# The bonus term of a linear-attention kernel as four 64x64 matmul tiles, with its results in other PSUM banks

## The reference

```python
for t in range(S):
    kt, vt, rt, wt = (k[:, :, t], v[:, :, t], r[:, :, t], w[:, :, t])
    cur = np.einsum('bhd,bhe->bhde', u[None] * kt, vt)
    y[:, :, t] = np.einsum('bhd,bhde->bhe', rt, state + cur)
    state = wt[:, :, :, None] * state + np.einsum('bhd,bhe->bhde', kt, vt)
```

## Time and profile before

| what | value |
|---|---|
| median of 3 runs | 313.41 us |
| the profiled execution: its time, its span | 313.47 us, 311.8 us |
| TensorE matmul busy | 306.1 us, 98% of the span |
| VectorE, ScalarE, GpSimd busy | 199.5, 160.8, 110.7 us |
| granted TensorE clock, mean | 0.999 |
| chain that ended last, TensorE's share | 98% |

### The profile page before, as it was taken

How to read it: one execution, slowest core, us unless ns; L and a number is a source line. 1 busy time by engine, 2 the same in 40 slices (tenths; PEclk the granted TensorE clock), 3 DMA queues, 4 the chain that set the end, 5 groups by cost and what they waited for, 6 DMA issues and landing times.

```text
span 311.8 us, 7335 instructions
## 1 busy us (share of the span) xinstructions
PE 306.1 (98%) x2882; PEld 290.0 (93%) x2882; DVE 199.5 (64%) x349; ACT 160.8 (52%) x335; POOL 110.7 (35%) x107
## 2 busy tenths in 40 slices
PE   8989999999999999999999999999999999999996
PEld 3779999999999999999999998999999989999995
DVE  6979998987996989688151469936437265034332
ACT  6469877854676567457656937652113045311100
POOL 7450350038056416613700605741331058122310
PEclk9999999999999999999999999999999999999999
DMA  7999008107205503200052371000000300000012
GB/s 231 401 394 403 19 19 329 44 20 275 97 6 192 186 10 105 99 1 3 9 180 81 90 252 64 2 0 0 3 0 31 124 0 0 2 0 0 2 50 101
DMA packets 11176, 29.82 MB, mean 96 GB/s; under 512 B 1216, under 2 KB 5888, under 8 KB 9856
## 3 DMA queue, kind: packets, MB, share of 16 engines
q1 hardware_dynamic: 10720, 28.85, 25.3%
q10 hardware_dynamic: 416, 0.45, 0.4%
HBM read 26.45 MB, written 2.36 MB: 92 GB/s over the span
## 4 chain that ended last, share of the span: by engine, by line
PE 98%; DVE 1%; ACT 0%; issue 0%; DVEq 0%; ACTq 0%
PE dense L946 40%; PE dense L379 5%; PE dense L378 5%; PE dense L377 5%; PE puy L379 3%; PE puy L378 3%; PE ps L378 3%; PE ps L377 3%; PE puy L377 3%; PE ps L379 3%; PE dense L373 2%; PE ps L782 2%; PE puy L896 2%; PE puy L872 2%; PE puy L851 2%; PE pkt L379 2%
## 5 line engine op out<-in xcount | busy, mean ns | idle before, releaser
L676 POOL TENSOR_TENSOR k_l<-sq,k_h 128x512 fp32r<-128x512 f32 x22 | 29.2, 1331 | 33.5 <-ACT sq L1262 27.1
L946 PE MATMUL dense<-xkr_h,wk_h 128*128 128x256 f32 x144 | 38.5, 289 | 0.0
L946 PE MATMUL dense<-k_h,wv_h 128*128 128x256 f32 x144 | 38.4, 288 | 0.0
L946 PE MATMUL dense<-k_h,wv_l 128*128 128x256 f32 x144 | 36.5, 283 | 0.0
L946 PE MATMUL dense<-xkr_h,wk_l 128*128 128x256 f32 x144 | 36.2, 283 | 0.0
L946 PE MATMUL dense<-k_l,wv_h 128*128 128x256 f32 x144 | 32.9, 283 | 0.0
L743 POOL TENSOR_TENSOR gated_l<-gf,gated_h 128x384 fp32r<-128x384 f32 x16 | 16.2, 1011 | 46.4 <-ACT gated_h L1411 36.4
L946 PE MATMUL dense<-xkr_l,wk_h 128*128 128x256 f32 x144 | 30.4, 283 | 0.0
L1411 ACT CAST gated_h<-gf 128x384 fp32r<-128x384 f32 x16 | 8.2, 515 | 42.9 <-DVE gf L1816 42.9
L946 PEld LDWEIGHTS dense<-xkr_h,wk_h 128*128 128x128 f32 x144 | 27.5, 191 | 0.3
L946 PEld LDWEIGHTS dense<-k_h,wv_h 128*128 128x128 f32 x144 | 27.0, 192 | 0.4
(11 more groups left out here) (256 smaller groups left out, 905.3 us busy)
## 6 DMA issues: line engine op xcount, KB each, us to landing
inw<-in_units SPq DMA_DIRECT2D x10, 1026.5 KB, 4.8
vb<-in_vT SPq DMA_DIRECT2D x12, 384.0 KB, 6.8
wsg_raw<-in_wsgT SPq DMA_DIRECT2D x1, 2304.0 KB, 9.9
out_y<-y_out SPq DMA_DIRECT2D x12, 192.0 KB, 1.9
wk_raw<-in_moe_w_k SPq DMA_DIRECT2D x3, 512.0 KB, 10.0
wv_raw<-in_moe_w_v SPq DMA_DIRECT2D x4, 384.0 KB, 15.7
win_raw<-in_moe_w_in SPq DMA_DIRECT2D x3, 512.0 KB, 4.2
inw<-in_units SPq DMA_DIRECT2D x2, 512.0 KB, 5.1
```

Source lines behind the costliest of these rows:

```text
L676: pool.tensor_tensor(k2_l[:, 2 * n:2 * n + 2], sq[:, j % 2].rearrange("p (g t) -> p g t", g=2), k2_h[:, 2 * n:2 * n + 2], ALU.subtract).th ...
L946: return pe.matmul(pm[bk][:, n * T:(n + 1) * T], weight[:, t, cols], inputs[:, t], start=first, stop=last, skip_group_check=True)
```

## The change

All units get their bonus in one way. A pair's two heads are two matmuls of 64 rows and 64 output columns, so that a unit's bonus is 8 float32 matmuls (16 passes) in the four 64x64 tiles of the array, in the order in which `from_state` uses them. Pairs 0 and 1 go to one bank and pairs 2 and 3 to another: `pu` and `py` for unit 0, `pm[0]` and `pm[1]` for unit 2, `pm[0]` and `pm[2]` for unit 3, and the first 256 columns of both score banks `ps` for unit 1 and units 4 to 11. The products by u on GpSimd, the rounding on ScalarE (six copies and the eight that made the matrix of ones) and the rest on GpSimd are gone. The waits follow the banks:

```diff
+        def bonus_place(un):
+            if un == 0:
+                return puy[:, :, STATE:2 * STATE]
+            if un in (2, 3):
+                return dense[:, 0:un:un - 1, 0:STATE]
+            return ps[:, :, 0:STATE]
...
-            return [ps[:, 0, 0:C], pkt[:, 0:C]][un] if un in MOVED else y_bank(un)[:, MAIN:WIDE]
+            return pkt[:, 0:C] if un == 1 else y_bank(un)[:, MAIN:WIDE]
...
             def scores(un):
                 pe.wait_ge(att_done, un)
-                pe.wait_ge(bonus_done, 2)
+                pe.wait_ge(bonus_done, 2 if un < 5 else un)
...
             def keys_by_step(un):
                 if un:
-                    pe.wait_ge(bonus_done, un)
+                    pe.wait_ge(y_done, 2)
...
             def bonus(un):
                 pe.wait_ge(rkp_done, un + 1)
-                if un == 1:
+                if un == 0:
+                    pe.wait_ge(flag_done, 1)
+                elif un == 1:
                     pe.wait_ge(att_done, 1)
+                elif un == 2:
+                    emptied(pe, ("k", 0, KS[1][1]))
+                    emptied(pe, ("k", 0, KS[2][1]))
                 elif un == 3:
+                    pe.wait_ge(bonus_done, 3)
                     emptied(pe, ("k", 0, KS[3][1]))
-                elif un:
-                    pe.wait_ge(ktok_done, states(un + 1))
-                    pe.wait_ge(bonus_done, un)
-                if un >= WIDE_FROM:
...
-                for g in range(PAIRS):
-                    cols = slice(g * C, (g + 1) * C)
-                    mm = pe.matmul(bonus_bank(un)[:, cols], u_b[:, g], rkp[:, un % 2, cols], start=True, stop=True)
+                else:
+                    pe.wait_ge(att_done, un + 1)
+                for n in range(PAIRS // 2):
+                    for part in range(2):
+                        g = n + part * PAIRS // 2
+                        for h in range(2):
+                            head = slice(h * SLOT, (h + 1) * SLOT)
+                            mm = pe.matmul(bonus_place(un)[slot(g, h), part, n * C:(n + 1) * C], u_b[head, g, slot(g, h)],
+                                           rkp[head, un % 2, g * C:(g + 1) * C], start=True, stop=True)
                 mm.then_inc(c_mm, 1)
...
+                if (kind, xs) == VS[0] and s == 0:
+                    pe.wait_ge(bonus_done, 4)
...
             def bonus(un):
                 dve.wait_ge(c_mm, un + 1)
+                if un == 0:
+                    dve.wait_ge(u_mm, 1)
...
                 elif s == 1:
-                    scan(b)
+                    scan_on(b)
+                    scan_back(b)
                     mask(a)
+                    queries(b)
                     bonus(a)
```

More of the change, by code:

```diff
@@ L94, in build @@
         k_in, e = put("k_in", e, [2, WIDE])
-        rk_at = e
         rkp, e = put("rkp", e, [2, WIDE])
-        rk_l, _ = put("rk_l", rk_at, [2, WIDE], FR)
         k_tok, e = put("k_tok", e, [2, PAIRS, P])
@@ L104, in build @@
         y3, e = put("y3", e, [2, C])
-        moves, _ = put("moves", e, [KT, P])
-        rk_h, e = put("rk_h", e, [2, WIDE], FR)
-        heads, e = put("heads", e, [2, P], FR)
+        moves, e = put("moves", e, [KT, P])
         junk, e = put("junk", e, [PAIRS, C])
@@ L183, in build @@
         x2, e = put("x2", r3, [KT, B * S])
-        U_COL = PAIRS * P
-        MU = U_COL + PAIRS
+        MU = PAIRS * P
         par, e = put("par", e, [MU + 2 * KT + GT])
-        u_b = par[:, 0:U_COL].rearrange("p (g e) -> p g e", g=PAIRS)
-        u_col = par[:, U_COL:MU]
+        u_b = par[:, 0:MU].rearrange("p (g e) -> p g e", g=PAIRS)
         mu = par[:, MU:MU + 2 * KT].rearrange("p (n t) -> p n t", n=2)
@@ L218, in build @@
         MOVED = range(N)
-        def bonus_bank(un):
-            return [py, ps[:, 1]][un] if un < N else pm[2] if un == 3 else pkt[:]
+        def bonus_place(un):
[4 more added lines that the diff above has]
+            return ps[:, :, 0:STATE]
         def score_banks(un):
@@ L261, in build @@
             "prod_done", "inv_done", "suffix_done", "rkp_done", "rin_done", "kin_done"))
-        rku_done, rkh_done, rkl_done, heads_done = (sem(n) for n in ("rku_done", "rkh_done", "rkl_done", "heads_done"))
         c_mm, kt_mm, sc_mm, u_mm, y_mm, flag_mm, last_mm, moved_mm = (sem(n) for n in (
@@ L341, in build @@
         BY_SCALAR = [(N * s + 1, 1) for s in (1, 2)]
-        WIDE_FROM = 3 * N
         def given(eng, s):
@@ L643, in products @@
             def products(un):
-                if un < 4:
-                    pool.wait_ge(rin_done, un + 1)
+                if un < 2:
+                    pool.wait_ge(s_rk[un], 16)
                 else:
@@ L680, in _ @@
             products(0)
+            pool.wait_ge(rin_done, 2)
             products(1)
@@ L692, in _ @@
                 key_low(0, n)
-            pool.wait_ge(rin_done, 6)
+            pool.wait_ge(kin_done, 6)
             products(5)
@@ L699, in _ @@
                 key_low(1, n)
-            weighted(6)
+            products(6)
             key_low(1, KG - 1)
-            weighted_low(6)
             for s in range(2, STAGES):
@@ L705, in _ @@
                 if b < NU:
-                    weighted(b)
-                    weighted_low(b)
+                    pool.wait_ge(rin_done, b + 1)
+                    products(b)
                 for n in range(KG):
@@ L710, in _ @@
                 if a + 2 < NU:
-                    weighted(a + 2)
-                    weighted_low(a + 2)
+                    pool.wait_ge(rin_done, a + 3)
+                    products(a + 2)
             def power(n):
@@ L1171, in keys @@
                 act.copy(k_tok[:, j % 2].rearrange("p g d -> p (g d)"), pkt[:]).then_inc(ktok_done, 1)
[L1173 to L1185, removed]
             def carry(un):
@@ L1331, in _ @@
                     hand_on(act, b, 1)
-                    weighted_high(b + 1)
                     mix(s + 1)
@@ L1340, in _ @@
                     key_high(s, 0)
-                    weighted_high(b)
                     keys(b)
@@ L1550, in bonus @@
             def bonus(un):
-                values = inw[:, un % 3, VF]
+                values = inw[:, un % 3, VF].rearrange("p (b n) -> p b n", b=2)
                 dve.wait_ge(c_mm, un + 1)
+                if un == 0:
+                    dve.wait_ge(u_mm, 1)
                 if un < 2:
                     dve.wait_ge(s_vf[un], 16)
-                dve.tensor_tensor(values, bonus_bank(un), values, ALU.mult).then_inc(bonus_done, 1)
+                dve.tensor_tensor(values, bonus_place(un), values, ALU.mult).then_inc(bonus_done, 1)
             added = pu[:, 0:STATE].rearrange("p (g e) -> p g e", g=PAIRS)
@@ L1852, in lay_out @@
     u_b = _np.zeros((P, PAIRS, P), _np.float32)
-    u_col = _np.zeros((P, PAIRS), _np.float32)
     for g in range(PAIRS):
@@ L1858, in lay_out @@
             u_b[rows, g, half * SLOT:(half + 1) * SLOT] = u[2 * g + h][:, None]
-            u_col[rows, g] = u[2 * g + h]
     order = []
@@ L1869, in lay_out @@
     arrays["vT"] = _np.concatenate(vT, axis=1)
-    arrays["params"] = _np.concatenate([u_b.reshape(P, PAIRS * P), u_col, *by_row], axis=1)
+    arrays["params"] = _np.concatenate([u_b.reshape(P, PAIRS * P), *by_row], axis=1)
     arrays["moe_w_k"] = inputs["moe_w_k"][order]
```

17 lines of the change are left out of this document (removed).

## The result

The changed kernel is slower: 314.12 us median of 17 runs (313.77 to 314.74) against 313.43 (313.23 to 313.58, 17 runs), a ratio of 1.0023 with a 95% interval from 1.0016 to 1.0030. The profiled execution took 314.74 us (span 313.0); it is the slowest of the 17. Its trace is compared with the earlier trace rows at places where TensorE starts the same work; the difference of the two start times I call the lag (positive is later than before).

The account below looks back on a forecast made before the run. TensorE, busy 306.1 of 311.8 us, was taken as the bound. Unit terms -0.44 - 0.29 - 0.44 + 0.48 + 0.26 - 0.40 = -0.83 us, from 313.47 to 312.64, gave a forecast of 312.6 us, range 311.8 to 313.4.

Parts of the forecast that it names:

- Unit 1, -0.44: Start-up: bonus starts at 14.68 as before, takes 0.69 instead of 1.13 us, and all of stage 0 moves forward: -0.44 us.
- rival B: No difference: unit 1's gain of 0.44 us does not come through the start-up, 313.1 us; chance 0.17.
- Units 0 and 2, 0: Each bonus 0.29 us shorter, but lost at waits for GpSimd's product (unit 0) and r_in (unit 2): 0.
- Unit 3, 0: Bonus 0.4 to 0.5 us shorter, but lost because the first half of its outputs waits for its mask: 0.
- Unit 4, -0.29: Bonus on TensorE's path drops from 0.89 to 0.60 us: -0.29 us.
- Unit 11, -0.40: Bonus and following half drop from 0.68 + 0.49 to 0.44 + 0.33 us: -0.40 us.
- Units 6 to 9, +0.48: Bonus rises from 0.48 to 0.60 us in each of four units, with no new wait for VectorE: +0.48 us.
- Unit 5, -0.44: Bonus and from_state 0.60 us shorter, less a 0.16 us wait for VectorE's read before unit 6's scores: -0.44 us.
- Unit 10, +0.26: Bonus plus from_state -0.04 us, plus a 0.30 us wait for VectorE's read before unit 11's scores: +0.26 us.
- Work taken from GpSimd and ScalarE, 0: Products, casts and copies removed where TensorE never waits for these engines, so worth 0.
- Rival A: Slower: scores wait for VectorE's read of the bonus in units 4 to 10, not only 5 and 10: 314.1 us; chance 0.08.
- three things that I had named as proof against myself: Dense layer of stage 0 not about 0.45 us earlier; gap before scores of units 7 to 10; bonus far from 0.60.

Follow-up runs that it names:

- a_shift: Changed kernel with 96 empty instructions ahead of TensorE's program, which the build removed, so the changed kernel itself once more: 314.10 us.
- h_4_5_11: Kernel before with the new bonus in units 4, 5 and 11 alone: 312.55 us, ratio 0.9966.
- h_6_10: Kernel before with the new bonus in units 6 to 10 alone: 314.13 us, ratio 1.0019.
- h_3: Kernel before with the new bonus in unit 3 alone: 313.63 us, ratio 1.0003.
- a_order: a_old_2_3 with one line moved, so that TensorE's scores name the wait for VectorE's read of the bonus first instead of fourth: 312.69 us.
- h_0_1_4_5_11: Kernel before with the new bonus in units 0, 1, 4, 5 and 11: 312.02 us, ratio 0.9951.
- a_old_2_3: Changed kernel with units 2 and 3 back in the old full-array form: 312.93 us, ratio 0.9980.
- a_params: Changed kernel with four unused zero columns, making the parameter array as wide as in the kernel before: 314.21 us.
- a_free: Changed kernel with the bonus of units 5 and 10 in two other banks, so the next scores need not wait for VectorE's read: 313.81 us.
- h_plus64: h_4_5_11 with 64 more TensorE instructions at the very start (one warming matmul replaced by 17 tiny ones): 317.67 us.

## Why the prediction was wrong

Forecast 312.6, measured 314.12, outside the range. The step that failed: the sum moves TensorE's chain by what each bonus and each wait changes and takes everything between them as unchanged, the first v tile of stage 1 too. That tile cost 0.99 us (a_shift) to 1.27 us (the first profile) more, because TensorE waited in it for its own code. Step by step, by the profiles:

- **Unit 1, -0.44:** right. The eight profiles with the new start-up have their first dense tile at 20.30 to 20.84 us, mean 20.49; the four with the old one (before, h_4_5_11, h_6_10, h_3) at 20.74 to 20.96, mean 20.88: -0.39. Only the changed kernel's own profile, with its late transfer, shows -0.11, as rival B had it.
- **Units 0 and 2, 0:** right. **Unit 3, 0:** the wait for the mask is right; the halt inside the half costs 0.19.
- **Unit 4, -0.29:** -0.31. **Unit 11, -0.40:** -0.39. **Units 6 to 9, +0.48:** +0.45.
- **Unit 5, -0.44:** -0.23. The 0.60 behind the flag and the 0.44 of from_state are right. The wait before the scores was sized with 0.10 us for the semaphore, taken from the wait for r_in in unit 3; here it is 0.26, since two more steps of waiting stood behind this one (a_order); that is 0.16 of the 0.21. **Unit 10, +0.26:** +0.44, for the same reason.
- **Work taken from GpSimd and ScalarE, 0:** nothing in the runs contradicts it.
- **The v tile of stage 1, taken as 0:** TensorE's own code was missing as a resource. I counted the passes of each bonus in time and never in instructions. The changed kernel has 228 more of TensorE's records, 96 of them ahead of the first v tile of stage 1. This moved a block's border from past that tile to behind its 16th pass (behind the 30th in h_0_1_4_5_11 and a_old_2_3), close behind the densest stretch of small matmuls (the outputs of unit 5 and the scores of unit 6), where the next block isn't there yet. In the first profile this cost 1.27 us (lag -0.46 to +0.81), of which 1.02 is the standstill; in a_shift the standstill is 0.74 and the tile 0.99 longer.

For the profiled execution the terms make -0.11 + 0.19 - 0.31 - 0.23 + 1.27 + 0.45 + 0.44 - 0.39 = +1.31, measured +1.27. With the usual start-up it is 0.3 less, and with a shorter standstill less again, which is where the median of +0.69 lies; how long the standstill is in runs without a profile, nobody sees. Of the forecast's miss of 1.5 us about 1.0 is the code, 0.2 the half of unit 3 and 0.4 the two waits; by the first profile alone the code would be 1.3, and the parts make 0.3 more than the medians' miss. Rival A had nearly the right time (314.1) with the wrong mechanism: no wait stands before the scores of units 7 to 10. Of the three things that I had named as proof against myself, a gap before those scores and a bonus far from 0.60 did not occur. The third, a first dense layer that doesn't start about 0.45 us earlier, occurred in the first profile (0.11) and not in the later ones (0.41 to 0.65 before the 20.95 of the kernel before, but for a_order with 0.36); it pointed at a transfer that was late once, not at the cause. None of the signs could have pointed at code.

Open: why the block for this border is asked for late (its packet starts at 72.86 to 73.18 us in the first profile, a_shift, a_params and a_free, when 233 to 243 of the 256 records of the block before it have begun; in the kernel before it is 139), whether other transfers delay it, and what happens in the 1.3 us between its landing and the next pass.

## What to carry to other kernels

Replacing few wide matmuls by many small ones has a price beyond its passes: count TensorE's instructions, and look at what follows a dense stretch of small matmuls; idle time that no engine explains, that stands at the same pass in several profiles and moves when instructions are added elsewhere, is a candidate for code: set it against the packets of the instruction queue. Test a change unit by unit, since units whose own gain is nothing can turn the sign. And name the wait that comes last in time so that it sits on the instruction itself: here one line took 0.20 us off each of two waits.

## What the runs showed of the hardware

- TensorE went on 1.26 to 1.36 us after its block's packet had landed, in all five profiles with the standstill; no border in any of the 14 profiles was passed sooner after its packet.
- A wait that leaves 0.20 us of idle time in the page cost about 0.4 (a_free): a pass takes 0.2 to 0.3 us from start to end, while groups of four passes of small tiles start 0.11 us apart, and idle time counts from the last end.
- From the end of VectorE's read to the first pass: 0.06 us where the wait sits on the weight load, 0.26 where it is followed by others (a_order, a_old_2_3).
- Float32 passes of 32 columns started 0.11 us apart at a granted clock of 1.00 and 0.21 us apart at 0.50 (h_plus64). The clock fell in the midst of these passes, at 8.03 us.
